# Second layer as two stages of seven block products each, its activations kept in DRAM between them

## The reference, cut to what matters

```python
kv = einsum('bhsd,bhse->bhde', k, v)            # 8 batches, 8 heads, 576 x 64
o = einsum('bhsd,bhde->bhse', q, kv)
x = rmsnorm(o) * g_norm                         # -> 4608 tokens x 512
x = (sigmoid(x @ w_gate) * (x @ w_val)) @ w_out # 512 -> 1536 -> 512
h = x @ w_in                                    # second layer, 512 -> 2048
g = where(h >= 1, h, where(h <= -1, 0, (h + 1) ** 2 / 4))
return g @ w_out2                               # 2048 -> 512
```

## Time and profile before

| what | value |
|---|---|
| median of the runs | 1785.83 us |
| lowest and highest run | 1779.93 and 1786.36 us |
| span of the profiled execution | 1778.6 us |
| TensorE (PE) busy | 1768.4 us, 99% |
| VectorE (DVE) busy | 700.6 us, 39% |
| ScalarE (ACT) busy | 590.7 us, 33% |
| GpSimd (POOL) busy | 129.8 us, 7% |

### The profile page before, as it was taken

How to read it: one execution, slowest core, us unless ns; L and a number is a source line. 1 busy time by engine, 2 the same in 40 slices (tenths; PEclk the granted TensorE clock), 3 DMA queues, 4 the chain that set the end, 5 groups by cost and what they waited for, 6 DMA issues and landing times.

```text
span 1778.6 us, 20275 instructions
## 1 busy us (share of the span) xinstructions
PE 1768.4 (99%) x7942; PEld 1458.4 (82%) x7944; DVE 700.6 (39%) x910; ACT 590.7 (33%) x897; POOL 129.8 (7%) x151
## 2 busy tenths in 40 slices
PE   9999999999999999999999999999999999999999
PEld 5888888888888888888888788888888888888887
DVE  2343433525344343443511444444434443434343
ACT  4452433424234242333423322232223232323222
POOL 4650000000000000000036200000000000000000
PEclk9999999999999999999999999999999999999999
DMA  5432020020201102010033201010101010101000
GB/s 189 122 95 92 4 91 15 27 77 15 80 15 50 53 15 91 3 51 1 1 95 95 78 1 48 1 48 1 47 0 47 0 47 0 47 0 48 1 24 24
DMA packets 30509, 77.18 MB, mean 43 GB/s; under 512 B 7808, under 2 KB 8832, under 8 KB 29312
## 3 DMA queue, kind: packets, MB, share of 16 engines
q1 hardware_dynamic: 25024, 58.73, 9.9%
q0 software_dynamic: 5440, 17.83, 3.4%
HBM read 56.62 MB, written 19.92 MB: 43 GB/s over the span
## 4 chain that ended last, share of the span: by engine, by line
PE 99%; DVE 0%; DMA 0%; issue 0%; ACT 0%; ACTq 0%; DVEq 0%
PE mid L678 18%; PE mid L680 18%; PE mid L679 18%; PE acc L678 13%; PE acc L680 13%; PE acc L679 13%; PE att L694 2%; PE mid L788 1%; PE ms L718 0%; PE ms L719 0%; PE ms L731 0%; PE att L679 0%; PE att L678 0%; PE att L680 0%; DMA ring<-kv_in 0%; DVE a_lo L530 0%
## 5 line engine op out<-in xcount | busy, mean ns | idle before, releaser
L678 PE MATMUL mid<-a_hi,w_lo 128*128 128x512 f32 x1184 | 461.6, 390 | 1.2 <-DVE a_lo L530 1.2
L679 PE MATMUL mid<-a_lo,w_hi 128*128 128x512 f32 x1184 | 460.6, 389 | 0.0
L680 PE MATMUL mid<-a_hi,w_hi 128*128 128x512 f32 x1184 | 460.6, 389 | 0.0
L595 DVE TENSOR_TENSOR h_raw<-mid,gate 128x512 f32<-128x512 f32 x108 | 74.6, 691 | 489.5 <-PE mid L680 456.5
L678 PEld LDWEIGHTS mid<-a_hi,w_lo 128*128 128x128 f32 x1184 | 222.3, 188 | 48.1 <-DVE a_lo L530 2.1
L680 PEld LDWEIGHTS mid<-a_hi,w_hi 128*128 128x128 f32 x1184 | 222.3, 188 | 46.0
L679 PEld LDWEIGHTS mid<-a_lo,w_hi 128*128 128x128 f32 x1184 | 222.3, 188 | 45.9
L503 ACT ACTIVATE gate<-h_raw,half_col 128x512 f32<-128x512 f32 x144 | 104.1, 723 | 447.1 <-DVE h_raw L652 447.1
L678 PE MATMUL acc<-w_hi,h_lo 128*128 128x512 f32 x576 | 224.3, 389 | 1.9 <-issue 1.0
L679 PE MATMUL acc<-w_lo,h_hi 128*128 128x512 f32 x576 | 224.1, 389 | 0.0
L680 PE MATMUL acc<-w_hi,h_hi 128*128 128x512 f32 x576 | 224.1, 389 | 0.0
(11 more groups left out here) (98 smaller groups left out, 1775.0 us busy)
## 6 DMA issues: line engine op xcount, KB each, us to landing
w_raw<-w_in POOLq DMA_DIRECT2D x68, 256.0 KB, 2.9
ring<-kv_in SPq DMA_DIRECT2D x30, 512.0 KB, 3.6
y_scratch<-x_raw SPq DMA_DIRECT2D x36, 256.0 KB, 2.8
ring<-y_scratch SPq DMA_DIRECT2D x9, 1024.0 KB, 5.3
out<-x_raw SPq DMA_DIRECT2D x36, 256.0 KB, 2.1
ring<-q_in SPq DMA_DIRECT2D x15, 512.0 KB, 3.7
ring<-kv_in SPq DMA_DIRECT2D x8, 256.0 KB, 3.6
x_raw<-kv_in SPq DMA_DIRECT2D x2, 512.0 KB, 7.2
```

What stands on the lines that cost most here:

```text
L595: nc.vector.tensor_tensor(h_raw[:], mid[1][:], gate[:], ALU.mult).then_inc(h_raw_ready, 1)
L678: nc.tensor.matmul(dst, s_lo, m_hi, start=start, stop=False)
L679: nc.tensor.matmul(dst, s_hi, m_lo, start=False, stop=False)
L680: return nc.tensor.matmul(dst, s_hi, m_hi, start=False, stop=stop)
```

## The change

The token and feature axes of each matrix of the second layer are cut in two, and the 2 x 2 block product is done with seven products in place of eight, by sums and differences of blocks (operands) before and of products after. It is done for the two matrix products one after the other.

First stage (`in_product`): 8 blocks of 576 tokens, 8 weight sets each, so 64 steps. A step has seven products of 6 matmuls with 288 moving columns: 2688 matmuls. After a step VectorE and ScalarE combine the products to four result blocks of 288 columns (c11, c12, c21, c22 in `c_tile`; three intermediate products are first copied out of PSUM by ScalarE: `p1_kept`, `u2_kept`, `u3_kept`), clamp, square and maximum work on all four at once (1152 columns), and SP stores them to `g_scratch` in DRAM. The seven token operands ("items", 128 x 576 each) are made once per block, from one load of 1.2 MB, split into high and low. The first `c11` of VectorE waits until all outputs of the first layer are stored.

Second stage (`out_product`): 18 units of 256 tokens, each with seven products of 24 matmuls with 256 moving columns: 3024 matmuls. Here the activations are loaded back (2 MB per unit), summed, and split, seven items of 128 x 1024 per unit.

The weights of both stages come as 32 "halves". GpSimd loads a half with two DMAs of 128 KB (`load_half`), makes four sums or differences of 128 x 128 (`sum_half`), ScalarE casts the seven blocks of it (128 x 896) and VectorE makes the low parts. Halves 0 to 15 belong to the first stage, 16 to 31 to the second.

The core of it, GpSimd first:

```diff
+            load_half(0)
+            load_half(1)
+            for i in range(2 * HALF_SETS):          # 32 halves
+                sum_half(i)
+                if 1 <= i < 2 * HALF_SETS - 1:
+                    pool.wait_ge(v_ready, i)
+                    load_half(i + 1)
+            def sum_half(i):
+                pool.wait_ge(stage_loaded[i % 2], 32 * (i // 2 + 1))
+                if i < HALF_SETS:
+                    nc.gpsimd.tensor_tensor(st[4], st[2], st[3], ALU.add).then_inc(stage_summed, 1)
+                    nc.gpsimd.tensor_tensor(st[2], st[0], st[2], ALU.subtract).then_inc(stage_summed, 1)
...
+            def load_half(i):
+                for a in range(2):
+                    pool.dma_start(stage[:, i % 2, 2 * a:2 * a + 2, :], src[:, :, P * h:P * (h + 1)])...
```

ScalarE and VectorE in tile 8 of the first layer (`hook` runs at the end of step f), `split_half(i)` of ScalarE waiting for the four sums of half i, that of VectorE for ScalarE's cast:

```diff
+            def before_hidden(f):                   # ScalarE
+                if 4 <= f < 4 + ITEMS:
+                    split_item(0, f - 4)
+                if f >= 6:
+                    split_half(2 * (f - 6))
+                    split_half(2 * (f - 6) + 1)
+            def before_hidden(f):                   # VectorE
+                if 5 <= f < 5 + ITEMS:
+                    split_item(0, f - 5)
+                if f - 4 in (1, 2, 4, 5):
+                    sum_item(0, f - 4)
+                if f >= 7:
+                    split_half(2 * (f - 7))
+                    split_half(2 * (f - 7) + 1)
```

ScalarE in iteration k of the first stage (65 iterations; X, Y, Z are pairs of banks):

```diff
+                    act.wait_ge(p_done[1], k + 1)
+                    nc.scalar.copy(c_kept[:, 0, :], X[k % 2][:, 0:C]).then_inc(p1_kept, 1)
+                    act.wait_ge(p_done[4], k)
+                    nc.scalar.copy(c_tile[:, (k - 1) % 3, 2, :], X[(k - 1) % 2][:, 0:C]).then_inc(c21_ready, 1)
+                    act.wait_ge(p_done[6], k + 1)
+                    nc.scalar.copy(c_kept[:, U2_KEPT + k % 2, :], X[k % 2][:, 0:C]).then_inc(u2_kept, 1)
...
+                if k < 2:                            # halves 12 to 15
+                    split_half(HALF_SETS - 4 + 2 * k)
+                    split_half(HALF_SETS - 3 + 2 * k)
+                if STEPS - SETS + 2 <= k < STEPS:    # k = 58 to 63, halves 16 to 27
+                    q = k - (STEPS - SETS + 2)
+                    split_half(HALF_SETS + 2 * q)
+                    split_half(HALF_SETS + 2 * q + 1)
+                    act.wait_ge(clamp_ready, k)
+                    nc.scalar.activation(c_sq[:], c_sq[:], ACT.Square, ...)
+                    act.wait_ge(p_done[7], k + 1)
+                    nc.scalar.copy(c_kept[:, U3_KEPT, :], X[k % 2][:, 0:C]).then_inc(u3_kept, 1)
+                if k == STEPS - 1:                   # halves 28, 29
...
+            split_half(2 * HALF_SETS - 2)
+            split_half(2 * HALF_SETS - 1)
```

```diff
+                    dve.wait_ge(u3_kept, k)
+                    nc.vector.tensor_tensor(c_tile[:, (k - 1) % 3, 3, :], Y[...][:, 0:C], c_kept[:, U3_KEPT, :], ALU.add)
+                    dve.wait_ge(p_done[3], k)
+                    nc.vector.tensor_tensor(c_tile[:, (k - 1) % 3, 1, :], Y[...][:, 0:C], c_kept[:, ...], ALU.add)
+                    nc.vector.tensor_scalar(c_sq[:], c_tile[:, (k - 1) % 3, :, :], 1.0, -1.0, ALU.min, ALU.max)
...
+                    dve.wait_ge(square_ready, k)
+                    nc.vector.tensor_tensor(c_tile[...], c_tile[...], c_sq[:], ALU.max).then_inc(g_ready, 1)
```

TensorE in iteration k, and the second stage:

```diff
+            for k in range(STEPS + 1):
+                    in_product(k, 1, X, True)
+                    in_product(k, 5, Y, True)
+                    pe.wait_ge(u3_kept, k)
+                    in_product(k - 1, 4, X, False)
+                    pe.wait_ge(p1_kept, k + 1)
+                    in_product(k, 6, X, False)
+                    pe.wait_ge(c22_ready, k)
+                    in_product(k - 1, 3, Y, False)
+                    in_product(k, 2, Z, True)
+                    pe.wait_ge(u2_kept, k + 1)
+                    in_product(k, 7, X, False)
...
+            for u in range(UNITS):
+                out_product(u, 1, X, True)          # u == 0 waits for all 32 halves
...
```

More of the change, by code:

```diff
@@ new lines, in store_unit @@
+            def store_unit(u):
+                for ready in (c11_ready, c12_ready, c21_ready, c22_ready):
+                    sp.wait_ge(ready, STEPS + u + 1)
+                for i in range(2):
+                    sp.dma_start(out[u // 2, 2 * (u % 2) + i, :, :], o_tile[:, u % 2, i, :]).then_inc(out_stored[u % 2], 16)
+            sp.wait_ge(a_ready, K * TILES)
+            load_block(0)
+            store_y(TILES - 1)
+            for b in range(BLOCKS):
+                sp.wait_ge(t_ready, ITEMS * (b + 1))
+                if b < BLOCKS - 1:
+                    load_block(b + 1)
+                else:
+                    hidden_stored(sp, STEPS - SETS)
+                    load_unit(0)
+                for s in range(SETS):
+                    store_hidden(SETS * b + s)
@@ L424, in tile, with split_half @@
-            def tile(t, n_kind="full", weights=None):
+            def split_half(i):
+                q, h = divmod(i, 2)
+                act.wait_ge(stage_summed, 4 * (i + 1))
+                if i < HALF_SETS:
+                    last_unit = (4 * (D_SLOTS * 8 * ROWS + ITEMS * 2 * P * (q + 1)) - 1) // (4 * N)
+                    act.wait_ge(h_used, K * (S1 * (TILES - 1) + min((last_unit + 1) // 3, S1)))
+                else:
+                    act.wait_ge(p_done[3], STEPS - SETS + q - SETS + 1)
+                nc.scalar.copy(v_hi[:, q % SETS, :, P * h:P * (h + 1)], stage[:, i % 2, :, :]).then_inc(v_hi_done, 1)
@@ L483, in _ @@
             tile(TILES - 2, "rest")
[L484 to L495, removed]
@@ L588, in tile @@
+            def tile(t, n_kind="full", hook=None):
                 n = t + 1
@@ L866, in _, with seven @@
-            tile2(0, False)
-            pe.wait_ge(w_ready, U1 + U2)
-            with nc.Fori(1, TILES - 2, 2, engines=(mybir.EngineType.PE,), hint_back_edge=True) as t:
-                tile2(t, True)
-                tile2(t + 1, False)
-            tile2(TILES - 2, True)
-            tile2(TILES - 1, False)
-            out_chunk2(TILES - 1, S2 - 1)
+            def seven(dst, width, step, number, terms, start):
+                for n, (s_hi, s_lo, m_hi, m_lo) in enumerate(terms):
+                    first, last = n == 0, n == len(terms) - 1
+                    nc.tensor.matmul(dst[:, 0:width], s_lo, m_hi, start=start and first, stop=False, skip_group_check=True)
+                    nc.tensor.matmul(dst[:, 0:width], s_hi, m_lo, start=False, stop=False, skip_group_check=True)
+                    done = nc.tensor.matmul(dst[:, 0:width], s_hi, m_hi, start=False, stop=last, skip_group_check=True)
+                done.then_inc(p_done[number], 1)
@@ new lines, in in_product @@
+            def in_product(k, number, dst, start):
+                b, s = divmod(k, SETS)
+                i = ITEM_IN.index(number)
+                hi, lo = t_slot(ITEMS * b + i)
+                if s == 0:
+                    pe.wait_ge(t_ready, ITEMS * b + i + 1)
+                if number == 1 and b == 0:
+                    pe.wait_ge(v_ready, 2 * k + 2)
+                quad = QUAD_IN[number]
+                terms = [(v_hi[:, s, quad, P * c:P * (c + 1)], v_lo[:, s, quad, P * c:P * (c + 1)], hi[:, c, :], lo[:, c, :])
+                         for c in range(2)]
+                seven(dst[k % 2], C, k, number, terms, start)
@@ new lines, in out_product @@
+            def out_product(u, number, dst, start):
+                i = ITEM_OUT.index(number)
+                hi, lo = s_slot(ITEMS * u + i)
+                pe.wait_ge(s_ready, ITEMS * u + i + 1)
+                quad = QUAD_OUT[number]
+                if u == 0 and number == 1:
+                    pe.wait_ge(v_ready, 2 * HALF_SETS)
+                terms = [(hi[:, j, :], lo[:, j, :], v_hi[:, j, quad, :], v_lo[:, j, quad, :]) for j in range(SETS)]
+                seven(dst[u % 2], R, STEPS + u, number, terms, start)
```

582 lines of the change are left out of this document (401 added, 181 removed).

## The result

The changed kernel takes 1854.24 us (median of 4 runs, 1852.84 to 1855.52) against 1785.85 us (the three runs of the kernel before and a fourth, 1785.87): a ratio of 1.0396, 95% interval 1.0378 to 1.0414. It is slower by 68 us; the forecast was 1837 us, with a range of 1765 to 1880. The profiled execution has a span of 1851.0 us, forecast 1829.6; it is that of the fastest of the four, 1852.84.

A forecast was written before the change was run, and what follows sets the result against it. TensorE's matmuls were taken to bound the kernel before. To its 1778.6 us span: -98 columns, +74 start, +55 end, +12 steps, rest clock and edges, giving 1829.6; with 7.2 for timed runs, 1837 us, range 1765 to 1880.

The forecast's parts named there:

- The halves decide: GpSimd loads and sums weight halves strictly in order, so TensorE idles at the first stage's start and end; forecast chance 0.58.
- 74 + 55 = 129 us: TensorE time lost to the halves: 74 us at the first stage's start, 55 us at its end.
- the 29 that I had put: First stage's end: time the rest of the 64 steps would take while the last halves are prepared, 29 us.
- the middle: First stage between its two gaps: 56 steps to iteration 58 at 5.58 us plus 2.0, ending at 1392.1.
- One half, 5.88 us: GpSimd's cycle per half: issue 0.30 and 0.54, landing 2.9, four sums 2.08 plus 0.06; ends 4.3 and 6.5.
- The step, 5.57: Normal first-stage step as a chain through product 3, c12, clamp, square and products 4, 6, 3: 5.57 us, against TensorE's 5.36.
- the shadow of the square: First stage: VectorE's item work, 11 x 0.76 us per block of 8 steps, fits beside the square and product 3.
- The clamp, 0.75: First-stage clamp over 1152 elements within SBUF, priced like a memset at 0.75 us; 1.37 at the general rate.
- Rival (b): Clamp runs at the general rate, VectorE and ScalarE become the first stage's loop: 36 us more, 1873; chance 0.12.
- The matmuls by columns: Second layer's matmul time goes by columns, 0.1275 and 0.1133 us each: 685 us in all, 98 us less.
- rival (c): Matmul surplus is paid per matmul: 20 us in the second stage, 6 in the loop, 1863; chance 0.14.
- rival (a): Weight halves keep up with TensorE; 1708 us if nothing of them shows; chance 0.16, mostly as half-times of 3.5 to 4.5.

The follow-up runs named there:

- three free runs: Changed kernel without GpSimd's loads and sums for all halves, halves 0 to 15, or halves 16 to 31: 1747.81, 1784.34 and 1820.71 us.
- free_all: Changed kernel with GpSimd's loads and sums of all 32 weight halves left out, casts and low parts kept: 1747.81 us.
- clamp_twice: Changed kernel with every clamp of the first stage made twice, one after the other: 1906.89 us.
- pace: Separate kernel of matmuls only, 48 per width and type, new stationary operand each: 0.226 us for 512 fp32r columns, 0.119 for 256.
- presum_same: Changed kernel with all halves summed in the first layer and stored in DRAM, low parts in the casts' step: 1763.55 us, 0.9892 of the kernel before.
- presum_tuned: presum_same with the last two halves' casts and last four low parts moved into iteration 64: 1759.55 us, 0.9883 of the kernel before.

## Why the prediction was right, and where its sum was off

- **The halves decide: right.** The forecast put the first load at 953.7, measured 952.73; the last gap's first load at 1397.2, measured 1399.03; the second stage at 1481.8, measured 1482.45. The three free runs show the cause and its size. That size was forecast as 74 + 55 = 129 us, while taking the halves away gave 106.4. Between the traces of the changed kernel and free_all the start differs by 72 us, close to the 74; it is the end that was mis-sized, 35 us for 55. Even with free halves the rest of the first stage takes 48 us from there (in free_all from 1328.2, the same place of the same step, to 1376.42) and not the 29 that I had put: six steps of 6.48, and the turn between the stages with its waits of 6.8 and 6.2.
- **That the second stage's start came within 0.7 us is luck in part.** The start was 8.8 us early, the middle 10.6 longer, the end 1.2 shorter, and these cancel.
- **One half, 5.88 us: 5.31 measured.** The sums came 0.42 apart, not 0.52 (-0.4 over four); the price by two memsets was too high. The rest, 3.74 to the first sum, was 3.54. The fourteen half-times of the start, each 0.57 less, are 8.0 of the 8.8 us by which it came early (1068.85 instead of 1077.6). At the end the forecast held only since the distance there is 5.69. The 4.9 us by which its 13 distances exceed 5.31 each are, in the trace, five slow sums (0.81 to 1.07 us in place of 0.45, 2.4 us in all), two loads issued late (1.7) and one that landed late (1.1). Of all 128 sums 12 took more than 0.55 us, up to 1.58, and during each of these 12 VectorE was at an instruction within SBUF; of the other 116, 102 had no VectorE instruction beside them, and six had one within SBUF and stayed below 0.55. So the slow sums go with VectorE's work; no run changed that work alone. The estimate of 0.51 us per sum that I had worked out from the Trainium skill (GPSIMD Engine Reference, section Elementwise — side-by-side cycle accounting) is above the 0.45 measured for the first sixteen.
- **The step, 5.57: 5.65 measured**, and every eighth 6.26, 5.74 on the mean of 53 steps. 18 matmuls at 0.1333 in place of 0.1275 are the +0.1. The +0.6 of every eighth step goes with VectorE's item work of a new block (TensorE waits 0.38 us for `tb_lo` at 1205.99, and its restart adds the 0.17 or so that I had allowed for one), which I had put into the shadow of the square. Together 56 x 0.16 = 9 of the 10.6 us by which the middle was longer.
- **The clamp, 0.75: 0.767.** Rival (b) fell, and clamp_twice shows that at the general rate it would indeed have cost its difference in every normal step. The rule that one-source fp32 work within SBUF moves two elements per cycle (the Trainium skill, VectorE: DVE Perf Modes, section The perf-mode tier table) agrees: 0.767 us for 1152 elements, against 1.358 for the maximum with two sources.
- **The matmuls by columns: wrong, the mis-sized term.** The second stage was 3024 x 0.1133 = 342.6; it is 3024 x 0.1200 = 362.9, and these 20 us are nearly all of the 21.4 by which the span was missed. I argued that narrow matmuls at 0.111 show no surplus. pace shows that they couldn't: 0.111 is a floor that 224 and 128 columns share, so it says nothing of columns (that it is the load of the stationary operand is argued, not tried), and from 256 on the 13 ns come on top of the columns. The earlier trace rows alone can't tell the two readings apart; rival (c) had the right one and was given 0.14.
- **Why seven for eight gives so little even when free.** By columns the second layer was to save 98 us. Free halves save 35: the surplus is paid on 2256 more matmuls (30 us), the steps are 0.14 longer than their matmuls (9), and the rest (24) is, as far as it was followed, the turn between the stages, its last steps (6.48 us each, with ScalarE and VectorE at the halves) and the ends. So rival (a)'s 1708 us for halves that keep up was 40 too low, and its bound of 4.1 us per half, below which the change gains, too high: with 28 half-times in the path, coming down from 1854 to 1782 us takes 2.6 us off each, so the bound is about 3 us (an estimate).
- The profiled span misses by 21.4 and the forecast time by 17, since the median lies 3.2 us above this span, where I took 7.2. On record every run's time is 1.8 us above its own span; the rest of both figures is that the median and the profiled run are different executions.

## What to carry to other kernels

Count a saving on TensorE in matmuls as well as in columns: at 256 columns of fp32r the surplus of 13 ns is 12% on top of the columns, at 512 it is 6%, and here the surplus of the added matmuls took back 30 of the 98 us that eight-to-seven saves in columns. Before an in-order engine is put into a chain, write down its cycle (load, wait, work, release) and compare it with the time that the consumer leaves; an engine that is 10% busy can hold TensorE for a hundred microseconds. Work on constants, such as sums of weights, belongs in a stretch where its engine is idle and nothing is queued behind it: this, with the low parts made a step earlier, turned 4% slower into 1.1 to 1.4% faster. And when two variants differ by a few us, line their traces up at a place behind the start-up before comparing them: here the start-up alone scattered by up to 5.7 us.

## What the runs showed of the hardware

- fp32r matmuls cost their columns at 2.4 GHz plus 12 to 13 ns each, and not less than 0.111 us at 224 and 128 columns with a new stationary operand; bf16 at 512 columns has 2 ns. At the lower clock no surplus is seen: 0.24 us for 288 columns is what they take at 1.2 GHz.
- TensorE came back at 1.2 GHz after idle times of 12.79 us (0.24 apart from 1069.25, until 1072.6) and 8.82 us (0.213 apart, until 1485.6).
- A sum of fp32 on GpSimd takes 1.3 us at 512 columns, 0.45 at 128 and 0.19 at 8. At 128 columns it took 0.68 to 1.58 us in 12 of 128 cases, all of them beside VectorE work within SBUF. Its two loads of 128 KB in a row keep it for 1.44 us and land in 2.7; one of 448 KB lands in 3.8 (presum_same) to 4.2 (presum_tuned).
